# Moving the highs of the second dense step's w1, one x copy and one queue wait, and adding filler matmuls between the first two attention units

## What is computed

```python
kv = np.einsum('bhsd,bhse->bhde', k, v)                # 4 x 8 heads, 576 rows, 64 columns
out = np.einsum('bhsd,bhde->bhse', q, kv)
x = out / np.sqrt(np.mean(out * out, -1, keepdims=True) + 1e-06) * g_norm   # then 2304 x 512
...
for e in range(4):                                     # dense: D = 512, F = 1024
    out += p[:, e:e + 1] * (np.maximum(x @ w1[e], 0.0) @ w2[e])
...
for e in range(8):                                     # routed: one expert for each row
    out[mask] = gate_w[mask, None] * (np.maximum(x[mask] @ w1[e], 0.0) @ w2[e])
```

## Time and profile before

| | us |
|---|---|
| median of 3 runs | 1155.61 (1155.38 to 1157.05) |
| the profiled execution | 1154.58 |
| its span | 1153.0 |
| TensorE busy in the span (PE) | 1121.8 (97%) |
| VectorE, POOL, ScalarE busy | 730.4, 657.3, 454.7 |

### The profile page before, as it was taken

How to read it: one execution, slowest core, us unless ns; L and a number is a source line. 1 busy time by engine, 2 the same in 40 slices (tenths; PEclk the granted TensorE clock), 3 DMA queues, 4 the chain that set the end, 5 groups by cost and what they waited for, 6 DMA issues and landing times.

```text
span 1153.0 us, 18656 instructions
## 1 busy us (share of the span) xinstructions
PE 1121.8 (97%) x6184; PEld 988.4 (86%) x6185; DVE 730.4 (63%) x1160; ACT 454.7 (39%) x807; POOL 657.3 (57%) x609
## 2 busy tenths in 40 slices
PE   7989999999999999999999999999989999999996
PEld 7888999988889888988889888988977888888885
DVE  4877888888875878888875878888662222222221
ACT  4763444444534444444534444444322222222220
POOL 1577777799867777799857777777330111111101
PEclk9999999999999999999999999999999999999998
DMA  9936778777612349777612348777369849427960
GB/s 241 266 87 206 273 275 283 281 262 259 247 37 73 122 151 301 284 263 258 248 37 74 116 155 302 280 254 281 135 268 361 296 182 364 159 96 302 371 242 13
DMA packets 102433, 250.87 MB, mean 218 GB/s; under 512 B 8254, under 2 KB 48190, under 8 KB 94171
## 3 DMA queue, kind: packets, MB, share of 16 engines
q1 hardware_dynamic: 97360, 235.18, 59.0%
q0 software_dynamic: 4800, 14.72, 3.7%
q10 hardware_dynamic: 203, 0.05, 0.0%
HBM read 170.99 MB, written 79.98 MB: 218 GB/s over the span
## 4 chain that ended last, share of the span: by engine, by line
PE 81%; POOL 6%; DVE 4%; issue 3%; DMA 3%; ACT 1%; SPq 0%; POOLq 0%; DVEq 0%; ACTq 0%
PE ps L1258 25%; PE ps L1260 25%; PE ps L1259 25%; DMA w_raw<-in_moe_w_dram 2%; PE ps L1447 2%; POOL w_lo L482 1%; PE ps L1413 1%; DMA q<-in_q_dram 1%; PE ps L1351 1%; DVE x_rows L953 1%; POOL w_lo L477 1%; DVE hT_lo L942 1%; POOL x_ops_lo L515 1%; DVE ahead_lo L961 0%; PE ps L1215 0%
## 5 line engine op out<-in xcount | busy, mean ns | idle before, releaser
L1258 PE MATMUL ps<-x_ops_hi,w_hi 128*128 128x384 f32 x672 | 226.4, 337 | 4.5 <-DVE sum L923 4.2
L1258 PE MATMUL ps<-w_hi,hT_hi 128*128 128x512 f32 x576 | 227.1, 394 | 2.1 <-DVE x_rows L951 2.1
L1260 PE MATMUL ps<-x_ops_hi,w_lo 128*128 128x384 f32 x672 | 225.7, 336 | 0.0
L1259 PE MATMUL ps<-x_ops_lo,w_hi 128*128 128x384 f32 x672 | 225.3, 335 | 0.0
L1260 PE MATMUL ps<-w_hi,hT_lo 128*128 128x512 f32 x576 | 225.3, 391 | 0.0
L1259 PE MATMUL ps<-w_lo,hT_hi 128*128 128x512 f32 x576 | 225.0, 391 | 0.0
L953 DVE SCALAR_TENSOR_TENSOR x_rows<-ps,dense_probs,x_rows 128x512 f32<-128x512 f32 x270 | 190.2, 739 | 23.0 <-PE ps L1260 23.0
L607 POOL DMA_INDIRECT out_dram<-y_rows,row_ids x22 | 22.6, 1026 | 236.3 <-DVE y_rows L1156 141.8
L491 POOL TENSOR_TENSOR w_lo<-w_raw,w_hi 128x512 fp32r<-128x512 f32 x96 | 149.0, 1572 | 8.0 <-ACT w_hi L694 8.0
L1146 DVE TENSOR_TENSOR rhT_lo<-ps,rhT_hi 128x512 fp32r<-128x512 f32 x44 | 28.5, 686 | 172.0 <-ACT rhT_hi L814 172.0
L1258 PEld LDWEIGHTS ps<-x_ops_hi,w_hi 128*128 128x128 f32 x672 | 126.1, 188 | 10.0 <-DVE sum L923 6.2
(11 more groups left out here) (198 smaller groups left out, 2004.2 us busy)
## 6 DMA issues: line engine op xcount, KB each, us to landing
w_slots<-split_parts SPq DMA_DIRECT2D x64, 1024.0 KB, 5.7
w_raw<-in_moe_w_dram SPq DMA_DIRECT2D x96, 512.0 KB, 3.6
ahead_raw<-in_moe_w_dram SPq DMA_DIRECT2D x64, 512.0 KB, 6.7
split_parts<-ahead_hi SPq DMA_DIRECT2D x64, 512.0 KB, 5.5
split_parts<-ahead_lo SPq DMA_DIRECT2D x64, 512.0 KB, 6.2
row_tile<-dispatched_rows POOLq DMA_DIRECT2D x20, 257.0 KB, 5.7
kv<-in_k_dram SPq DMA_DIRECT2D x16, 288.0 KB, 7.5
kv<-in_v_dram SPq DMA_DIRECT2D x16, 288.0 KB, 8.6
```

The costliest lines, as they stand in the source:

```text
L1258: mm(out_, ah, bh, start=(first and m == 0), stop=False, skip_group_check=not final or not first)
L1259: mm(out_, ah, bl, start=False, stop=False, skip_group_check=not final or not first)
L1260: last = mm(out_, al, bh, start=False, stop=(final and m == n - 1), skip_group_check=not final or not first)
```

## The change

Five edits. (1) `X_ON_ACT` goes from 13 to 12: x of unit 12 is copied by ScalarE. (2) `w1_highs` is cut in two, `w1_raw_highs` and `w1_sum_highs`. For step 1 the raw half runs at the end of unit 14 and the sum half behind the last square, ahead of `root(15)`; from step 2 on both run where they did. (3) `write_x(14)` goes behind `copy_p1(0)`. (4) SP's wait for all of x moves from ahead of the steps to ahead of step 0's ahead loads. (5) 8 filler matmuls (`2 * WARM // 3`) run ahead of unit 1's products and 3 (`WARM // 4`) between its kv products and its q transposes.

```diff
-    X_ON_ACT = 13
+    X_ON_ACT = 12
...
             sp.wait_ge(w1_split, 1)
             load_w1(1)
-            sp.wait_ge(x_out, UNITS)
             for k in range(STEPS):
...
                 if k == 0:
+
+                    sp.wait_ge(x_out, UNITS)
                     for s in range(2):
                         load_ahead(s)
                     fill_rows()
...
-            def w1_highs(k):
+            def w1_sum_highs(k):
+                s = k % 2
+                act.wait_ge(w1_summed, 4 * k + 4)
+                A(w1h[s][:, 3:7].rearrange("p m c n -> p (m c n)"), tsum[:, :, :, :].rearrange("p m c n -> p (m c n)"), ACT.Copy).then_inc(w1_hi, 1)
+
+            def w1_raw_highs(k):
                 s = k % 2
                 act.wait_ge(w1_in, 16 * (k + 1))
                 if k >= 2:
...
                     act.wait_ge(xo_lo_pool, OPS)
                 A(w1h[s][:, 0:2], w1_raw4[:, :, :, 0:P], ACT.Copy).then_inc(w1_hi, 1)
                 A(w1h[s][:, 2], w1_block(1, 1), ACT.Copy).then_inc(w1_hi, 1)
-                act.wait_ge(w1_summed, 4 * k + 4)
-                A(w1h[s][:, 3:7].rearrange("p m c n -> p (m c n)"), tsum[:, :, :, :].rearrange("p m c n -> p (m c n)"), ACT.Copy).then_inc(w1_hi, 1)
+
+            def w1_highs(k):
+                w1_raw_highs(k)
+                w1_sum_highs(k)
...
                 if u == 6:
                     w1_highs(0)
+                if u == UNITS - 2:
+                    w1_raw_highs(1)
+            w1_sum_highs(1)
             root(UNITS - 1)
-            write_x(UNITS - 2)
...
                 copy_p1(k)
+                if k == 0:
+                    write_x(UNITS - 2)
...
-                if k + 1 < STEPS:
+                if 0 < k < STEPS - 1:
                     w1_highs(k + 1)
...
+            def fillers(n):
+                for _ in range(n):
+                    mm(ps[:, 7, 0:P], ident[:, :], ident[:, :], start=True, stop=True)
+
             def products_in(u, s, n_in):
 
+                if u == 1:
+                    fillers(2 * WARM // 3)
...
+                if u == 1:
+                    fillers(WARM // 4)
                 pe.wait_ge(q_in[s], n_in)
...
-            for _ in range(WARM):
-                mm(ps[:, 7, 0:P], ident[:, :], ident[:, :], start=True, stop=True)
+            fillers(WARM)
```

## The result

The changed kernel took **1151.5 us** (median of 8 runs, 1151.08 to 1154.24), the kernel before 1155.55 us beside it (8 runs, 1153.49 to 1157.76): a ratio of 0.9968, with a 95% interval of 0.9957 to 0.998. The profiled execution of the changed kernel took 1151.53 us, with a span of 1149.9 us for 1153.0.

A forecast was written before the change was run, and what follows sets the result against it. TensorE is almost always busy from 98.6 to 1040 us, so gains in its waits ahead of that should reach the end one for one. Terms 1.4 + 2.2 = 3.6 us off 1155.6 give 1152.0, range 1150.4 to 1155.2.

The forecast's parts named there:

- Part 1: Transposes of unit 13: with x(12) copied by ScalarE they start at 67.98 for 68.71, a gain of 0.73 us.
- Part 2: Moved highs and write_x(14): product 3 gains 1.2 us in dense step 0 and 1.4 us in step 1.
- Part 3: Inside step 0's down projection: earlier POOL lows and w1(2) load remove the 2.07 us wait for L951; 2.2 us gained.
- Part 4: Fillers around unit 1: unit 1 some 0.8 us later, all absorbed by later waiting; gain and cost put at 0.
- The lines on unit 5: TensorE's 1.53 us wait at 26.14 for v bytes covers the fillers and gets shorter by about 0.8 us.
- Only half: TensorE still finds combine(1) late, through POOL holding VectorE or ScalarE's order; 1.2 to 1.6 us won, 1154.2; chance 0.12.
- Fillers on the path: Fillers in attention aren't absorbed: 0.8 us of the gain go (1152.8), or 3.1 at half clock (1155.1); chance 0.09.
- Nothing: ScalarE's unit 15 or a wait elsewhere returns the gain, or it doesn't pass the routing: 1155.6; chance 0.09.
- Slower: w2(1) load lands late behind ahead loads and filler rows leaving SP right after it, holding ScalarE: 1157.9; chance 0.06.
- The rule that the prediction weighed: A two-SBUF-input VectorE instruction and a GpSimd instruction reading SBUF block each other for a whole instruction; not in the sum.

## Why the prediction was right

The forecast was 1152.0 us and the time 1151.5. The dates and waits ahead of `down(1)` came as forecast, so the mechanism is right. That the time came within 0.5 us is in part luck: two terms were right, a third was too large for a usual execution, the fourth was put at nothing, and the profile that the terms were read from was not a usual one.

**Part 1 was right.** 0.73 us were forecast at the transposes of unit 13, and 0.82 measured (1.27 less the 0.45 us by which unit 15's products, 63.16 for 63.61, were already early). `X_ON_ACT` alone gives the same 0.82.

**Part 2 was right**, in size and order: 1.2 us forecast at product 3 of step 0 and 1.31 measured beyond the 0.45; 1.4 us at step 1 and 1.33. The remaining wait was forecast at "some 0.4 us" and is 0.38. One sentence in it was only half of the truth. It says that VectorE is no longer the last ahead of product 3 of step 1; it was not, but the step does not name what is. The table load, in plain view on ScalarE, was worth 0.95 us there. The 0.2 us that were to come from a shorter L942 did not come: from product 3 of step 0 to that of step 1 the gain grows by 0.02.

**Part 3 had the right mechanism, and a size that holds only for a slow load.** Between the two profiles the term is 2.37 us for the 2.2 forecast. Each date of the chain came within a microsecond or so: POOL's lows at 68.7 for "near 70", the w1(2) load at 74.0 for 74.5, `down(1)` at 102.2 for 102.7, no wait left inside `down(0)`. The slack was 0.9 us for the half microsecond forecast (first add over at about 91.2, fifth tile at 92.14). Putting the highs back brought the wait back. But the forecast took the 2.07 us of one execution as the term, and of the four profiles with the highs in their old place its load was the slowest. With the load under way for 3.24, 3.51, 3.57 and 4.58 us, the wait was 0.85, 1.07, 1.06 and 2.07 us: to a tenth or so it follows the load one for one. So the step "the wait of 2.07 us goes, **2.2 us**" should have read 0.9 to 2.2. Where in that range a usual execution lies, four profiles can't say: in three it is 1.1 or less, but in the profiles with the load moved forward it takes 3.4 to 4.5 us. In intervals, old forms without the moved highs had 34.64 and 34.87 us for 35.88.

**Part 4 was wrong.** It says of the fillers that the clock is granted in full in 0 to 10 us, gap included, and "nothing here". The reading was right for that execution, and that execution was the exception: 0.996 mean granted clock where the kernel before otherwise had 0.988 to 0.995. The step that failed is the conclusion from one profile to the median of the runs, right next to the sentence that saw that the profiled execution was 1.0 us under the median. The column could not vouch for full clock there in any case: it reads 1.00 in the stretch in which the start's fillers are 0.21 us apart, twice the 0.11 of the later ones. The lines on unit 5 were right for this profile, where no wait is left; the two other profiles of the changed kernel still show 1.76 and 1.01 us. No run shows a cost of the eleven fillers.

The account by rows: 0.8 us (part 1), then 1.7 to 2.9 us of interval, by how fast the load is (34.64, 34.87 and 35.88 to 32.97), together 2.5 to 3.7, for 4.05, 4.05 and 4.8 us measured in three jobs. With the 1.3 us that the fillers brought on the kernel before and a fast load it comes to 3.8 to 4.0. **What stays open** is whether that last term belongs there, the fillers' worth on the changed kernel: everything but the fillers gained 4.4 and 3.9 us on the kernel before in its two jobs, as much as the whole sum. Without them it was 0.9 us slower in one job, but in the other it was no slower than the kernels with them (1151.83, at a granted clock of 0.991 to 0.993, beside 1152.3 with SP's wait put back, whose interval explains 0.36 of the difference). The half-clock stretch is shown; that what it costs reaches the end in the changed kernel is not.

**The rivals.** "Only half" did not come: no wait stands inside `down(0)` in any of the eight profiles that have the moved highs, the moved queue wait and the w2 load in its place. "Fillers on the path" did not: with them alone the kernel before was not slower. "Nothing" did not: the gain of `down(1)` stands at the routing, and the 1.1 us missing behind it are of one execution. "Slower" did not, since the w2 load landed in 4.0 us.

## What to carry to other kernels

A wait that hangs on a transfer has a length as uncertain as the transfer; before it goes into a sum at its full size, ask how fast the transfer has been elsewhere, and keep both ends. A stall named after one engine may belong to the copy or table load that stands ahead of its other operand: look at every operand's writer, in order, before calling the place finished. And compare the mean granted clock of the profiled execution with those of the other runs before reading "the clock is full here".

## What the hardware did that was not expected

**The clock falls in places of little idle time, and not each time, with the fillers too.** Beside the stretch at 12 us there were others deep in attention, in two of the ten profiles with fillers. In the kernel before with fillers, TensorE and its stretches of 2 us:

```profile
52.30 2.20 PE L1230 MATMUL ps<-kv_blocks,qT 128*96 128x128 f32 x10 [1.12 <-issue]
```
```profile
52.00:54.00 2.00, 1.70 (x9) 0.60 1.14 265
54.00:56.00 2.00, 2.00 (x28) 0.54 1.15 258
```

Ten matmuls took 2.20 us behind an idle time of 1.12 us; the changed kernel, whose idle time there was 0.57 us, took 1.25 us for the same ten. The length of that one idle time doesn't decide it: with the load of w2 late it was 1.40 us, and the ten took 1.25 us. In the changed kernel itself the clock fell twice in the execution of 1156.9 us, whose dense part starts at 74.17 us for 69.22. TensorE there (granted 0.50 from 30 to 32 us and 0.51 from 48 to 50; the same 12 matmuls take 1.48 us elsewhere):

```profile
27.90 0.92 PE L1218 MATMUL ps<-kv 96*64 96x64 f32 x24 [1.76 <-DMA kv<-in_v_dram]
...
30.76 2.51 PE L1235 MATMUL ps<-kv_blocks,qT 128*96 128x128 f32 x12
...
47.47 2.69 PE L1235 MATMUL ps<-kv_blocks,qT 128*96 128x128 f32 x12
```

So the clock stayed up at the hand-over of the first two units in all ten profiles with fillers, and not always behind it.

**A table load on an engine that is mostly idle was still on the path.** The load of 1.28 us at 79.68 cost TensorE 0.95 us, although ScalarE is busy for only 40% of the span. The Trainium skill, page "ScalarE: Activation LUTs", section "What ACT_TABLE_LOAD costs", gives about 1283 ns for the load, and some 1380 ns more for a drain. The first agrees with the rows here; of the second nothing is seen (the row behind the load starts 1.29 us after it, and one kernel's load starts at 81.97 where the activation ahead of it, 81.43 plus 0.53, ends).

**VectorE and POOL slow each other, in both directions.** Three of POOL's four sums of step 2 took 1.05 to 1.13 us in the changed kernel, beside VectorE's low parts, and 0.74 us before. Two of these low parts took 0.55 us all the same, the last one 0.88 us:

```profile
79.69 0.88 DVE L954 SCALAR_TENSOR_TENSOR hT_lo<-sum,hT_hi 128x384 fp32r<-128x384 f32 x1
```

Against POOL's larger operations that low part takes 1.64 us, as it did here before the change. The rule that the prediction weighed, of the Trainium skill, page "SBUF — State Buffer", section "Who interferes with whom", agrees with these rows. It spoke against the change and cost it nothing: POOL had the time, and the low part came out shorter.
